# A spatial product of 768 x 768 computed from seven block products instead of eight

## The chip, the core and the metric

The kernel runs on one core of one Trainium2 chip. Its metric is the device time in microseconds of one execution. The core's engines run side by side, each through its own list of instructions, and meet at semaphores: TensorE (PE) multiplies into PSUM, VectorE (DVE) and ScalarE (ACT) work elementwise on SBUF and PSUM, GpSimd (POOL) works on SBUF, and SyncE (SP) issues nearly all DMAs.

## What is computed

A retention layer feeds an MLP with a low-rank token mixing, and that feeds a spatially gated MLP. The change is in the last part. Batch B is 2, sequence S is 768, model width 512, and all data are 32-bit.

```python
def _moe2_ref(x, w_in, w_spatial, b_spatial, w_out) -> np.ndarray:
    h = np.maximum(x @ w_in, 0.0)
    d_ff = h.shape[-1]
    u, v = (h[..., :d_ff // 2], h[..., d_ff // 2:])
    mu = np.mean(v, axis=-1, keepdims=True)
    var = np.mean((v - mu) ** 2, axis=-1, keepdims=True)
    v_n = (v - mu) / np.sqrt(var + 1e-06)
    v_s = np.einsum('ts,bsd->btd', w_spatial, v_n) + b_spatial[None, :, None]
    gated = u * v_s
    return (gated @ w_out).astype(np.float32)
```

## The kernel before

**Precision.** A 32-bit operand of a matrix product is split in two: ACT rounds it to fp32r (`vh`, `wsph`, `gh`, `x2h`, `wouth`), and DVE or POOL forms the rest, operand minus rounded part (`vl`, `wspl`, `gl`, `x2l`, `woutl`). PE then makes three matmuls for each pair of tiles: high times high, high times rest, rest times high.

**Stages.** The retention part takes the first 67 us. Then come the 24 steps of the MLP, n = 0 to 23 (three token tiles of 512, each with eight steps). Its first product (`product`) already uses a scheme of seven block products q = 0 to 6: sums of blocks are multiplied, and results are put together from PSUM and three copies p1, p16 and p5. From the second token tile on, the input projection (`in_first`, `in_group`) of the tile before runs inside the steps. That of the last tile, t = 2, comes by itself at 367 to 389 us; it waits for `x2h` and `x2l`, made from `u`, to which DVE adds the MLP's result (L848). Groups 0 to 3 of a token tile give V (`vn`, normalised over its 512 channels on DVE at L869 with statistics from L859 and L863 and POOL's `rstd`, L446). Groups 4 to 7 give u.

**The spatial part** has eight pieces m, four tiles of 128 channels d in each of two batches. For each piece PE multiplies the six row tiles of V (stationary, 128x128) with the six row tiles of w_sp (moving, two halves of 384 columns), three matmuls each: 36. DVE adds the bias (L986), multiplies with u (L989) into `gt`, ACT rounds it to `gh` (L683) and DVE forms `gl` (L992). After a batch's four pieces the output projection (`out_proj`, L1280) multiplies the four tiles of `gh` and `gl` with `wouth` and `woutl`. Four banks hold its results, which ACT copies to `stage` (L688) and SP stores. PE waits at `wout_lo` before the first one.

**What sets the order.** Each engine's list is written by hand, loop by loop, as the functions below show, and an engine goes through its list strictly in order; SP's DMAs are in one queue too. A semaphore counts finished operations, for instance `sp_done` pieces of the spatial product.

## Time and profile before

| | us |
|---|---|
| median of 3 runs | 477.98 (476.96 to 478.22) |
| the profiled execution | 477.27 |
| its span | 475.4 |
| PE busy | 466.1 |
| DVE busy | 318.2 |
| ACT busy | 233.0 |
| POOL busy | 53.7 |

The span runs from the first to the last instruction; the 1.9 us around it are start and end. All times in rows are in microseconds from the span's start unless marked ns. In a row of a timeline, an "x4" behind several merged instructions gives their number and the second column their common length; the brackets hold how long the engine was idle before and what ended it. A duration includes the time until the result is written, so the next instruction of the same engine starts some 0.1 us before the end of the one before it. The matmuls of PE overlap too: a start-to-start distance is their cost in a row, and the duration is a latency.

### The profile page before, as it was taken

Reading aid. Unit: us, or ns where it says so; the run is one execution under the profiler, and the core shown is the slowest. Engines: PE = TensorE matmul, PEld = TensorE weight load, DVE = VectorE, ACT = ScalarE, POOL = GpSimd, SP = SyncE. Lnnn points to the kernel's source line nnn. Section 1 sums busy time; section 2 is a strip of 40 time slices with the busy share of each in tenths; the row PEclk is TensorE's granted clock in tenths of the full one; section 3 lists DMA queues with packets and bytes.
Section 4 is the critical chain, followed back from the end, with each engine's and each line's share of the span. In section 5 each row is a group of like instructions: output and inputs, shape, how many; then the busy total and the mean of one; then the engine's idle time right before and its main releaser. Section 6 shows DMA issues by size and latency. Waiting matters only on the chain.

```text
span 475.4 us, 8542 instructions
## 1 busy us (share of the span) xinstructions
PE 466.1 (98%) x3176; PEld 417.4 (88%) x3176; DVE 318.2 (67%) x697; ACT 233.0 (49%) x540; POOL 53.7 (11%) x56
## 2 busy tenths in 40 slices
PE   7999998999999999999999999999999999999997
PEld 4788887989999999888888998888888889999997
DVE  4788978888789988764765977765633684611630
ACT  1666745555667655643474555643333732222112
POOL 2278960000000000000100000001000050000000
PEclk9999999999999999999999999999999999999999
DMA  8999801362222342211220432220115200011003
GB/s 270 413 314 305 280 1 45 135 221 88 90 89 90 128 138 91 90 50 38 90 90 10 135 123 90 90 70 21 44 29 209 84 0 1 1 68 66 1 0 134
DMA packets 19929, 50.31 MB, mean 106 GB/s; under 512 B 1456, under 2 KB 3120, under 8 KB 18608
## 3 DMA queue, kind: packets, MB, share of 16 engines
q1 hardware_dynamic: 19472, 49.24, 29.9%
q10 hardware_dynamic: 416, 0.53, 0.4%
q8 instruction: 26, 0.43, 0.4%
q14 instruction: 15, 0.12, 0.1%
HBM read 46.61 MB, written 3.15 MB: 105 GB/s over the span
## 4 chain that ended last, share of the span: by engine, by line
PE 93%; DVE 2%; DMA 2%; ACT 1%; issue 1%; SPq 0%; DVEq 0%
PE bank L1265 11%; PE bank L1177 9%; PE bank L1175 9%; PE bank L1178 9%; PE bank L1158 8%; PE bank L1156 8%; PE bank L1159 8%; PE bank L1280 7%; PE bank L1217 2%; PE bank L1216 2%; PE bank L1215 2%; PE bank L1025 2%; PE bank L1070 2%; PE bank L1064 2%; DMA att<-attn 1%; PE bank L1210 1%
## 5 line engine op out<-in xcount | busy, mean ns | idle before, releaser
L1156 PE MATMUL bank<-bh,w1c 128*128 128x256 f32 x336 | 94.7, 282 | 2.2 <-DVE c L830 0.8
L1159 PE MATMUL bank<-bh,w1c 128*128 128x256 f32 x336 | 94.7, 282 | 0.0
L1158 PE MATMUL bank<-bl,w1c 128*128 128x256 f32 x336 | 94.6, 282 | 0.0
L1177 PE MATMUL bank<-hl,w2h 128*128 128x512 f32 x192 | 75.9, 396 | 0.0
L1175 PE MATMUL bank<-hh,w2h 128*128 128x512 f32 x192 | 75.8, 395 | 0.0
L1178 PE MATMUL bank<-hh,w2l 128*128 128x512 f32 x192 | 74.7, 389 | 0.0
L1156 PEld LDWEIGHTS bank<-bh,w1c 128*128 128x128 f32 x336 | 63.5, 189 | 9.2 <-DVE w1c L797 2.8
L1158 PEld LDWEIGHTS bank<-bl,w1c 128*128 128x128 f32 x336 | 63.4, 189 | 5.5
L830 DVE TENSOR_TENSOR c<-bank,p 128x256 f32<-128x256 f32 x72 | 30.5, 424 | 52.1 <-PE bank L1159 31.0
L1159 PEld LDWEIGHTS bank<-bh,w1c 128*128 128x128 f32 x336 | 63.4, 189 | 0.0
L549 ACT ACTIVATE p<-bank 128x256 f32<-128x256 f32 x72 | 27.5, 381 | 47.0 <-PE bank L1159 46.0
L1178 PEld LDWEIGHTS bank<-hh,w2l 128*128 128x128 f32 x192 | 36.1, 188 | 7.9
L564 ACT ACTIVATE hh<-c 128x256 fp32r<-128x256 f32 (+1 forms) x48 | 25.1, 523 | 30.8 <-DVE c L830 30.8
L1177 PEld LDWEIGHTS bank<-hl,w2h 128*128 128x128 f32 x192 | 36.6, 191 | 2.1
L524 ACT ACTIVATE w1c<-wsum 128x256 fp32r<-128x256 f32 x96 | 35.2, 410 | 6.6 <-DVE wsum L789 4.7
L1175 PEld LDWEIGHTS bank<-hh,w2h 128*128 128x128 f32 x192 | 36.2, 188 | 2.4
L797 DVE TENSOR_TENSOR w1c<-wsum,w1c 128x256 fp32r<-128x256 f32 x92 | 36.5, 417 | 0.0
L802 DVE TENSOR_TENSOR w2l<-w2raw,w2h 128x512 fp32r<-128x512 f32 x46 | 31.4, 683 | 7.2 <-ACT w2h L541 7.2
L444 POOL TENSOR_SCALAR vare<-mv 128x4 f32<-128x4 f32 x3 | 0.7, 226 | 314.0 <-DVE mv L863 314.0
L541 ACT ACTIVATE w2h<-w2raw 128x512 fp32r<-128x512 f32 x48 | 29.8, 620 | 0.0
L986 DVE TENSOR_TENSOR gt<-bank,bias_sb 128x384 f32<-128x384 f32 x16 | 8.2, 553 | 31.4 <-PE bank L1265 31.4
L524 ACT ACTIVATE w1c<-w1raw 128x256 fp32r<-128x256 f32 x72 | 26.8, 406 | 1.7 <-DMA w1raw<-w 1.7
(120 smaller groups left out, 904.4 us busy)
## 6 DMA issues: line engine op xcount, KB each, us to landing
w1raw<-w SPq DMA_DIRECT2D x24, 512.0 KB, 5.0
w2raw<-w SPq DMA_DIRECT2D x24, 512.0 KB, 4.0
att<-attn SPq DMA_DIRECT2D x7, 1152.0 KB, 7.2
att<-attn SPq DMA_DIRECT2D x10, 384.0 KB, 5.3
out_T<-stage SPq DMA_DIRECT2D x7, 384.0 KB, 2.3
wsp_raw<-w_sp SPq DMA_DIRECT2D x1, 2304.0 KB, 8.2
winraw<-w_in SPq DMA_DIRECT2D x1, 2048.0 KB, 9.4
tab<-decay SPq DMA_DIRECT2D x7, 258.0 KB, 4.2
```

The costliest lines, as they stand in the source:

```text
L524: nc.scalar.activation(w1c[k][:, 0, q, :], w_operand(k, q), ACT.Copy).then_inc(w1_hi, 1)
L797: nc.vector.tensor_tensor(w1c[k][:, 1, q, :], w_operand(k, q), raw(w1c[k])[:, 0, q, :], ALU.subtract).then_inc(w1_lo, 1)
L802: nc.vector.tensor_tensor(w2l[h][:, :], w2raw[n % 2][:, h, :], raw(w2h[h])[:, :], ALU.subtract).then_inc(w2_lo, 1)
L830: nc.vector.tensor_tensor(o, b, a[:, :], ALU.add).then_inc(c_sum, 1)
L1156: mm(o, w1c[k][:, 0, q, s], bh[:, q, c, :], start=(opens and c == 0), stop=False, skip_group_check=True)
L1158: mm(o, w1c[k][:, 0, q, s], bl[:, q, c, :], start=False, stop=False, skip_group_check=True)
L1159: m = mm(o, w1c[k][:, 1, q, s], bh[:, q, c, :], start=False, stop=(c == 1), skip_group_check=True)
L1175: mm(ch_ps[c][:, :], w2h[h][:, s], hh[k][:, h, :], start=(j == 0 and h == 0), stop=False, skip_group_check=True)
L1177: mm(ch_ps[c][:, :], w2h[h][:, s], hl[k][:, h, :], start=False, stop=False, skip_group_check=True)
L1178: m = mm(ch_ps[c][:, :], w2l[h][:, s], hh[k][:, h, :], start=False, stop=last, skip_group_check=True)
L1265: i = mm(o[h], w[m % 2][:, s, :], x[:, s, h * HS:(h + 1) * HS], start=(first and s == 0), stop=(last and s == NC - 1))
L1280: i = mm(o[h], w[:, d, s], x[:, d, h * HS:(h + 1) * HS], start=(first and d == 0), stop=(last and d == CT - 1))
```

## The change

**PE.** The eight pieces become four blocks a (two per batch), each of two d tiles by the whole token range. V^T and w_sp are split into two halves each way: the two d tiles, the two halves of the summed rows (three tiles of 128 each), and the two halves of 384 output columns. Seven products of three row tiles with three matmuls each make a block, 63 matmuls. The products go into bank x, z, x, y, x, y, x in the order of q, where x alternates between two banks from block to block. x and y are not opened by a matmul: ACT writes the bias, or the difference of its halves, into them first (`set_bias`).

**DVE** forms sums of blocks of w_sp (`sums_wsp`, four of 1152 columns, then seven rests) and of V (`sums_v`, four of 384 for each block, then seven rests). Per block it makes three result sums (`sum_sp`), four gates that write in place into u (`gate`), and four rests, in place too. The statistics of the last token tile move from behind `rest_v(1)` into block 1, and their normalisation behind block 1.

**ACT** rounds seven operands for each block and seven for w_sp, copies p1s, p16s and p5s out of PSUM, and writes the biases. The rounding of w_out moves into block 1.

**SP** loads the bias in MLP step 3, behind w_in, and w_out behind the input projection. `stage` holds one batch instead of two.

**POOL** keeps its list.

The diff, cut to the lists of ACT, DVE, SP and PE:

```diff
-        vs_ps, out_ps = [bank[0:2], bank[2:4]], bank[4:8]
+        x_ps, z_ps, y2_ps, out_ps = bank[2:4], bank[0], bank[4], (bank[1], bank[5], bank[6], bank[7])
...
                 if n == 3:
                     sp.wait_ge(u_done, 2 * NI)
                     sp.dma_start(winraw[:, :, :], w_in).then_inc(win_loaded, 16)
+                    sp.dma_start(bias_sb[:, :], bias).then_inc(bias_loaded, 16)
             sp.wait_ge(pr_done, NQ * NN)
             sp.dma_start(wsp_raw[:, :, :], w_sp).then_inc(wsp_loaded, 16)
-            sp.dma_start(bias_sb[:, :], bias).then_inc(wsp_loaded, 16)
-            sp.wait_ge(ch2_done, 2 * NN)
+            sp.wait_ge(in_done, 8 * NT)
             sp.dma_start(woutraw[:, :, :], w_out).then_inc(wout_loaded, 16)
...
+            def set_bias(a, i):
+                if i == 0:
+                    if a == 0:
+                        act.wait_ge(bias_loaded, 16)
+                        act.wait_ge(x2_sum, 4 * NT)
+                    elif a == 1:
+                        act.wait_ge(x2_sum, 4 * NT)
+                    else:
+                        act.wait_ge(gated, 4 * (a - 1))
+                    nc.scalar.activation(x_ps[a % 2][:, 0:HS], bias_sb[:, 0:HS], ACT.Copy).then_inc(bias_set, 1)
+                else:
+                    if a == 0:
+                        act.wait_ge(diff_done, 1)
+                        act.wait_ge(x2_sum, 4 * NT)
+                    else:
+                        act.wait_ge(sp_sum, 3 * a)
+                    nc.scalar.activation(y2_ps[:, 0:HS], bias_diff[:, :], ACT.Copy).then_inc(bias_set, 1)
...
+            for a in range(NA):
+                sp_copy(a, 0)
+                if a:
+                    set_bias(a, 1)
+                if a == 0:
+                    round_v(1, range(0, 2))
+                round_g(a, 0)
+                sp_copy(a, 1)
+                if a == 0:
+                    round_v(1, range(2, 4))
+                sp_copy(a, 2)
+                if a == 0:
+                    round_v(1, range(4, NQ))
+                elif a == 1:
+                    round_wout()
+                round_g(a, 1)
+                round_g(a, 2)
+                if a < NA - 1:
+                    set_bias(a + 1, 0)
+                round_g(a, 3)
+                if a == 1:
+                    round_v(2, range(NQ))
+                    out_copy(0, 0)
+                    out_copy(0, 1)
+                    round_v(3, range(NQ))
+                    out_copy(0, 2)
+                    out_copy(0, 3)
...
+            sums_v(0)
+            rest_v(0, range(0, 2))
+            add_x2(NT - 1, range(0, 3))
+            rest_v(0, range(2, 4))
+            add_x2(NT - 1, range(3, 4))
             rest_x2(NT - 1)
...
-            rest_v(0)
-            rest_v(1)
-            statistics(NT - 1, range(CT))
-            normalise(NT - 1)
-            dve.wait_ge(in_out, 8 * NT)
-            for m in range(CT * B):
-                gate(m)
-                if m + 2 < CT * B:
-                    rest_v(m + 2)
+            bias_difference()
+            sums_wsp()
+            rest_v(0, range(4, NQ))
+            rest_wsp(range(NQ))
+            sums_v(1)
+            for a in range(NA):
+                sum_sp(a, 0)
+                gate(a, 0)
+                if a == 0:
+                    rest_v(1, range(0, 2))
+                elif a == 1:
+                    statistics(NT - 1, range(CT))
+                rest_g(a, 0)
+                sum_sp(a, 1)
+                gate(a, 1)
+                if a == 0:
+                    rest_v(1, range(2, 4))
+                sum_sp(a, 2)
+                gate(a, 2)
+                rest_g(a, 1)
+                if a == 0:
+                    rest_v(1, range(4, NQ))
+                gate(a, 3)
+                rest_g(a, 2)
+                rest_g(a, 3)
+                if a == 1:
+                    normalise(NT - 1)
+                    sums_v(2)
+                    rest_v(2, range(NQ))
+                    sums_v(3)
+                    rest_v(3, range(NQ))
...
+            def spatial(a):
+                k, x, z, y = a % 2, x_ps[a % 2][:, 0:HS], z_ps[:, 0:HS], y2_ps[:, 0:HS]
+                for q in range(NQ):
+                    o = (x, z, x, y, x, y, x)[q]
+                    if a == 0:
+                        pe.wait_ge(wsp_lo, q + 1)
+                    pe.wait_ge(vl_done, NQ * a + q + 1)
+                    if q == 0:
+                        pe.wait_ge(bias_set, 2 * a + 1)
+                    if q == 1 and a:
+                        pe.wait_ge(sp_sum, 3 * (a - 1) + 1)
+                    if q == 2:
+                        pe.wait_ge(sp_copied, 3 * a + 1)
+                    if q == 3:
+                        pe.wait_ge(bias_set, 2 * a + 2)
+                    if q == 4:
+                        pe.wait_ge(sp_copied, 3 * a + 2)
+                    if q == 5:
+                        pe.wait_ge(sp_copied, 3 * a + 3)
+                    if q == 6:
+                        pe.wait_ge(sp_sum, 3 * a + 2)
+                    for s in range(NH):
+                        mm(o, vh[k][q][:, s, :], wsph[:, q, s, :], start=(q == 1 and s == 0), stop=False,
+                           skip_group_check=True)
+                        mm(o, vh[k][q][:, s, :], wspl(q)[:, s, :], start=False, stop=False, skip_group_check=True)
+                        m = mm(o, v_rest(a, q)[:, s, :], wsph[:, q, s, :], start=False, stop=(s == NH - 1),
+                               skip_group_check=True)
+                    m.then_inc(sp_done, 1)
```

In POOL's list nothing moves. In DVE's list the piece around the last additions to u read so before (`u<-bank,u` is the addition, `w2l` the rest of the last w2 tile):

```order
532 L802 TENSOR_TENSOR w2l_88<-w2raw_84,w2h_87 128x512 [waits w2_hi]
533 L848 TENSOR_TENSOR u<-bank,u 128x512 [waits ch_sum] x3
534 L848 TENSOR_TENSOR u<-bank,u 128x512 [waits ch2_done]
535 L853 TENSOR_TENSOR x2l<-u,x2h 128x512 [waits x2_hi] x4
536 L970 TENSOR_TENSOR wspl<-wsp_raw,wsph 128x768 [waits wsp_hi] x6
```

and reads so now (`vsum` are sums of blocks of V, `vn_rest` and `vsum_rest` rests):

```order
532 L940 TENSOR_TENSOR w2l_88<-w2raw_84,w2h_87 128x512 [waits w2_hi]
533 L1121 TENSOR_TENSOR vsum_119<-vn 128x384 [waits hid_lo,vn_done]
534 L1121 TENSOR_TENSOR vsum_119<-vsum_119,vn 128x384 [waits v_sum]
535 L1121 TENSOR_TENSOR vsum_119<-vn 128x384
536 L1121 TENSOR_TENSOR vsum_119<-vn,vsum_119 128x384 [waits v_sum]
537 L1128 TENSOR_TENSOR vn_rest<-vn,vh_0_122 128x3x128 [waits vh_done,v_sum]
538 L1128 TENSOR_TENSOR vn_rest<-vn,vh_1_123 128x3x128 [waits vh_done]
539 L986 TENSOR_TENSOR u<-bank,u 128x512 [waits ch_sum] x3
540 L1128 TENSOR_TENSOR vsum_rest_141<-vsum_119,vh_2_124 128x384 [waits vh_done]
541 L1128 TENSOR_TENSOR vsum_rest_141<-vsum_119,vh_3_125 128x384 [waits vh_done]
542 L986 TENSOR_TENSOR u<-bank,u 128x512 [waits ch2_done]
543 L991 TENSOR_TENSOR x2l<-u,x2h 128x512 [waits x2_hi] x4
```

Six operations on V stand ahead of the additions and two more ahead of the fourth. The statistics of the last token tile (BN_STATS), for which POOL's `rstd` and then `woutl` wait, stood ahead of the first gate (L986) in DVE's list:

```order
538 L976 TENSOR_TENSOR vl_116<-vn,vh_115 128x768 [waits vh_done]
539 L859 BN_STATS bnst<-vn 128x6 [waits in_out]
540 L863 BN_AGGR mv<-bnst 128x2 [waits vn_done,bn_done]
541 L859 BN_STATS bnst<-vn 128x6 [waits in_out]
542 L863 BN_AGGR mv<-bnst 128x2 [waits vn_done,bn_done]
543 L859 BN_STATS bnst<-vn 128x6 [waits in_out]
544 L863 BN_AGGR mv<-bnst 128x2 [waits vn_done,bn_done]
545 L859 BN_STATS bnst<-vn 128x6 [waits in_out]
546 L863 BN_AGGR mv<-bnst 128x2 [waits vn_done,bn_done]
547 L869 TENSOR_SCALAR vn<-vn,mv,rstd 128x512 [waits rstd_done]
548 L869 TENSOR_SCALAR vn<-vn,mv,rstd 128x512 x3
549 L986 TENSOR_TENSOR gt_120<-bank,bias_sb 128x384 [waits sp_done,in_out]
```

They now stand in block 1 (`csum` is a result sum, `u<-csum,u` a gate, `u_rest` its rest):

```order
579 L1172 TENSOR_TENSOR u<-csum_115,u 128x384 [waits sp_sum]
580 L997 BN_STATS bnst<-vn 128x6 [waits in_out]
581 L1001 BN_AGGR mv<-bnst 128x2 [waits vn_done,bn_done]
582 L997 BN_STATS bnst<-vn 128x6 [waits in_out]
583 L1001 BN_AGGR mv<-bnst 128x2 [waits vn_done,bn_done]
584 L997 BN_STATS bnst<-vn 128x6 [waits in_out]
585 L1001 BN_AGGR mv<-bnst 128x2 [waits vn_done,bn_done]
586 L997 BN_STATS bnst<-vn 128x6 [waits in_out]
587 L1001 BN_AGGR mv<-bnst 128x2 [waits vn_done,bn_done]
588 L1176 TENSOR_TENSOR u_rest<-u,gh 128x384 [waits gh_done]
589 L1161 TENSOR_TENSOR csum_114<-bank,p5s 128x384 [waits gated,sp_done,sp_copied]
590 L1172 TENSOR_TENSOR u<-csum_114,u 128x384 [waits sp_sum]
```

Eight rows of statistics stand between the gate and the rest of block 1's first quarter, behind the whole of block 0. ACT's list read so before, beside the first three pieces (`vh` a rounding of V, `gh` one of the gated tile):

```order
433 L678 ACTIVATE vh_113<-vn 128x768 [waits sp_done]
434 L683 ACTIVATE gh<-gt_120 128x768 [waits gated]
435 L678 ACTIVATE vh_115<-vn 128x768 [waits sp_done]
436 L683 ACTIVATE gh<-gt_121 128x768 [waits gated]
437 L678 ACTIVATE vh_113<-vn 128x768 [waits sp_done,vn_done]
```

The end of block 0 and the start of block 1 read now:

```order
451 L746 ACTIVATE vh_6_135<-vn 128x384
452 L786 ACTIVATE gh<-u 128x384 [waits gated] x2
453 L764 ACTIVATE bank<-bias_sb 128x384 [waits x2_sum]
454 L786 ACTIVATE gh<-u 128x384 [waits gated]
455 L780 ACTIVATE p1s<-bank 128x384 [waits sp_sum,sp_done]
456 L771 ACTIVATE bank<-bias_diff 128x384 [waits sp_sum]
457 L786 ACTIVATE gh<-u 128x384 [waits gated]
```

Row 453 writes the bias for block 1's first product. It stands behind the second and third rounding of the gated tile (L786) of block 0. Before, ACT wrote nothing that a spatial matmul's bank waited for.

## Rows read from the trace of the kernel before

**Rows 1.** The page: engine shares; granted clock in 40 slices, in tenths.

```profile
PE 466.1 (98%) x3176; PEld 417.4 (88%) x3176; DVE 318.2 (67%) x697; ACT 233.0 (49%) x540; POOL 53.7 (11%) x56
...
PEclk9999999999999999999999999999999999999999
```

**Rows 2.** The longest wait of PE in the table of waits; the chain in order.

```profile
PE bank L1103 <- DVE hh L714: 1.4, 1, 1.4
...
389.00 24.98 PE bank L1265 x144
413.99 16.66 PE bank L1280 x96
```

**Rows 3.** Timeline at the spatial part; groups of instructions (busy, mean ns).

```profile
388.84 0.51 PE L1265 MATMUL bank<-wsph,vh 128*128 128x384 f32 x2
...
401.54 1.02 DVE L986 TENSOR_TENSOR gt<-bank,bias_sb 128x384 f32<-128x384 f32 x2 [1.41 <-PE bank L1265]
...
L541 ACT ACTIVATE w2h<-w2raw 128x512 fp32r<-128x512 f32 x48 | 29.8, 620 | 0.0
...
L693 ACT ACTIVATE wsph<-wsp_raw 128x768 fp32r<-128x768 f32 x6 | 4.8, 836 | 0.0
L688 ACT ACTIVATE stage<-bank 128x384 f32<-128x384 f32 x16 | 7.1, 490 | 21.6 <-PE bank L1280 21.6
```

**Rows 4.** MLP step 3: SP's issue of w_in, its time to landing; ACT; PE.

```profile
89.62 0.60 SPq L362 DMA_DIRECT2D winraw<-w_in  x1
...
winraw<-w_in SPq DMA_DIRECT2D x1, 2048.0 KB, 9.4
...
100.34 0.72 ACT L524 ACTIVATE w1c<-w1raw 128x256 fp32r<-128x256 f32 x2 [1.70 <-DMA w1raw<-w]
100.97 0.36 ACT L549 ACTIVATE p<-bank 128x256 f32<-128x256 f32 x1
...
101.77 0.28 PE L1156 MATMUL bank<-bh,w1c 128*128 128x256 f32 x1
```

**Rows 5.** Timeline where the last input projection begins: DVE, ACT, PE.

```profile
362.90 0.69 DVE L802 TENSOR_TENSOR w2l<-w2raw,w2h 128x512 fp32r<-128x512 f32 x1 [7.18 <-ACT w2h L541]
365.15 2.73 DVE L848 TENSOR_TENSOR u<-bank,u 128x512 f32<-128x512 f32 x4 [1.56 <-PE bank L1178]
...
365.87 2.67 ACT L571 ACTIVATE x2h<-u 128x512 fp32r<-128x512 f32 x4 [3.01 <-DVE u L848]
371.72 0.60 ACT L577 ACTIVATE vn<-bank 128x512 f32<-128x512 f32 x1 [0.97 <-PE bank L1201]
...
366.99 0.39 PE L1194 MATMUL bank<-winh,x2h 128*128 128x512 f32 x1
...
372.71 0.39 PE L1211 MATMUL bank<-winl,x2h 128*128 128x512 f32 x1
```

**Rows 6.** Timeline of DVE and POOL from the last statistics to woutl.

```profile
381.27 0.69 DVE L859 BATCH_NORM_STATS2 bnst<-vn 128x6 f32<-128x512 f32 x1
...
384.37 0.18 DVE L863 BATCH_NORM_AGGREGATE mv<-bnst 128x2 f32<-128x6 f32 x1
386.03 5.80 DVE L869 TENSOR_SCALAR vn<-vn,mv,rstd 128x512 f32<-128x512 f32 x4 [1.47 <-POOL rstd L446]
...
384.95 1.04 POOL L446 TENSOR_TENSOR rstd<-vare,neg_half 128x4 f32<-128x4 f32 x1
385.96 5.58 POOL L469 TENSOR_TENSOR woutl<-woutraw,wouth 128x512 fp32r<-128x512 f32 x4
```

**Rows 7.** Timeline of POOL and DVE: a DVE operation alone and meeting POOL's.

```profile
55.85 2.52 POOL L429 TENSOR_TENSOR bl<-u,bh 128x512 fp32r<-128x512 f32 x2
58.33 1.87 POOL L429 TENSOR_TENSOR bl<-tsum_early,bh 128x512 fp32r<-128x512 f32 x1
...
57.34 1.72 DVE L752 TENSOR_TENSOR qd<-att,tab 128x640 f32<-128x640 f32 x1
...
13.30 0.83 DVE L752 TENSOR_TENSOR qd<-att,tab 128x640 f32<-128x640 f32 x1 [0.88 <-DMA tab<-decay]
```

More of the change, by code:

```diff
@@ L147, in retention_mlp_spatial_gating_kernel @@
-        woutraw, o = at("woutraw", W2_AT, [P, CT, C])
-        wouth, o = at("wouth", o, [P, CT, C], f32r)
-        woutl, o = at("woutl", o, [P, CT, C], f32r)
-        assert o <= C_AT
-        o = C_AT
-        for k in range(2):
-            gt[k], o = at(f"gt{k}", o, [P, S])
+        stage, o = at("stage", o, [P, CT, S])
+        wouth, o = at("wouth", o, [P, CT, C], f32r)
+        assert o <= VN_AT
+        woutraw, o = at("woutraw", VN_AT + 24 * KB, [P, CT, C])
+        p1s, o = at("p1s", o, [P, HS])
@@ new lines, in retention_mlp_spatial_gating_kernel @@
+        p16s, o = at("p16s", o, [P, HS])
+        p5s, o = at("p5s", o, [P, HS])
+        csum = [None, None]
+        for k in range(2):
+            csum[k], o = at(f"csum{k}", o, [P, HS])
+        assert o <= U_AT
+        wsp_raw, o = at("wsp_raw", B_AT, [P, NC, S])
+        wt, o = at("wt", o, [P, 4, NH, HS])
+        wsph, o = at("wsph", o, [P, NQ, NH, HS], f32r)
+        assert o <= W2R_AT
+        vsum, vh = [None, None], [[None] * NQ for _ in range(2)]
+        vsum[0], o = at("vsum0", C_AT, [P, 4, NH, P])
@@ L681, in round_g, with round_v @@
-            def round_g(m):
-                act.wait_ge(gated, m + 1)
-                nc.scalar.activation(gh[:, m % CT, :], gt[m % 2][:, :], ACT.Copy).then_inc(gh_done, 1)
+            def round_v(a, qs):
+                b, k = a // 2, a % 2
+                for q in qs:
+                    if q == 0:
+                        act.wait_ge(vn_done, CT * (b + 2))
+                        act.wait_ge(ch2_done, 2 * (NN - 1 + a) if a < 2 else 2 * NN)
+                    if q == 5 and a < 2:
+                        act.wait_ge(w2_lo, 2 * NN - 4 + 2 * a)
+                    if q in S_OF:
+                        act.wait_ge(v_sum, 4 * a + S_OF[q] + 1)
+                    if a >= 2:
+                        act.wait_ge(sp_done, NQ * (a - 2) + q + 1)
+                    nc.scalar.activation(vh[k][q][:, :, :], v_operand(a, q), ACT.Copy).then_inc(vh_done, 1)
@@ L685, in out_copy, with round_wout @@
+            def round_wout():
+                act.wait_ge(wout_loaded, 16)
+                for d in range(CT):
+                    nc.scalar.activation(wouth[:, d, :], woutraw[:, d, :], ACT.Copy).then_inc(wout_hi, 1)
             def out_copy(b, c):
+                if b:
+                    act.wait_ge(stage_free[c], 16)
                 for h in range(2):
                     act.wait_ge(out_done, 8 * b + 2 * c + h + 1)
-                    nc.scalar.activation(stage[:, c, b * S + h * HS:b * S + (h + 1) * HS],
+                    nc.scalar.activation(stage[:, c, h * HS:(h + 1) * HS],
@@ L701, in _ @@
[L701 to L709 removed]
+            round_v(0, range(NQ))
+            round_x2(NT - 1, range(CT))
+            set_bias(0, 0)
+            round_wsp(0)
+            round_wsp(1)
+            relu_in(NT - 1, range(0, 2))
@@ L712, in _ @@
+            for c in range(CT):
+                out_copy(1, c)
         @block.vector
@@ new lines, in sum_sp, with gate @@
+            def sum_sp(a, s):
+                copied, q, p, ps = ((1, 1, p1s, z_ps), (3, 4, p5s, x_ps[a % 2]), (2, 5, p16s, y2_ps))[s]
+                dve.wait_ge(sp_copied, 3 * a + copied)
+                dve.wait_ge(sp_done, NQ * a + q + 1)
+                k = 3 * a + s
+                if k >= 2:
+                    dve.wait_ge(gated, 4 * ((k - 2) // 3) + (k - 2) % 3 + 1)
+                nc.vector.tensor_tensor(csum[k % 2][:, :], ps[:, 0:HS], p[:, :], ALU.add).then_inc(sp_sum, 1)
+            def gate(a, s):
+                if s < 3:
+                    dve.wait_ge(sp_sum, 3 * a + s + 1)
+                    x = csum[(3 * a + s) % 2][:, :]
+                else:
+                    dve.wait_ge(sp_done, NQ * (a + 1))
+                    x = x_ps[a % 2][:, 0:HS]
+                if a == 0 and s == 0:
+                    dve.wait_ge(in_out, 8 * NT)
+                nc.vector.tensor_tensor(u_part(u, a, s), x, u_part(u, a, s), ALU.mult).then_inc(gated, 1)
@@ L1285, in _ @@
             for b in range(B):
-                for d in range(CT):
-                    spatial(CT * b + d)
+                spatial(2 * b)
+                spatial(2 * b + 1)
                 if b == 0:
```

225 lines of the change are left out of this document (142 added, 83 removed).

## The prediction

> **What bounds the kernel now.** I read the engine shares first: PE is busy for 98% of the span, at the full granted clock in all forty slices [rows 1]. So the question is whether PE's queue has holes where the change works. The chain in order of time says no: the first four spatial pieces are one unbroken run of 24.98 us, and the first output projection is one of 16.66 us right behind it [rows 2]. The longest wait of PE that the table of waits shows is 1.4 us, at the start [rows 2]. Here every matmul taken away is time gained and every wait put in is time lost, to the full.
>
> The spatial part is 288 matmuls of 384 columns. 144 of them are the run of 24.98 us [rows 2]: 0.1735 us each. From a last matmul's start to the start of DVE or ACT is 0.39 us: the run begins at 388.84, its 72nd matmul at 388.84 + 71 x 0.1735 = 401.16, DVE starts at 401.54 [rows 3].
>
> **What goes.** Four blocks of seven products of nine matmuls are 252 instead of 288. 36 x 0.1735 = **6.25 us less** on PE. Each matmul still has a weight load of its own before and after, and the single bank per product costs nothing: the last output matmuls and the MLP's products already accumulate into one.
>
> **What is added, by place.** For 384 columns I take on DVE 0.55 us to the end and 0.47 to the next start, from the pair of 1.02 us out of PSUM [rows 3]; 0.83 us for 640 columns in SBUF [rows 7] is the same rate. On ACT I take 0.52 and 0.42, between 0.49 out of PSUM and the line through 0.62 for 512 and 0.84 for 768 columns in SBUF [rows 3]. Wider ones go by the same slopes: 1152 columns cost DVE 1.27 and ACT 1.05. Waking PE costs 0.17 more: the copy freed its bank at 372.32 and the matmul that was due at 372.43 has its successor at 372.71 [rows 5].
>
> *1. The bias load, moved ahead of a weight load.* SP now issues it between w_in and the fifth w1 tile. That tile was the one DMA that ACT waited for (1.70 us, until 100.34), with the copy p16 queued behind it on ACT; the copy ended at 101.33 and PE's fifth product started at 101.77 [rows 4]. So the cover is 101.77 - 101.33 - 0.17 = 0.27 us. w_in landed at 89.62 + 9.4 = 99.0 and the tile's 512 KB behind it at 100.3, so 384 KB more are 1.0 us: PE stands for 1.0 - 0.27 = **0.75 us** (0.3 if the DMA engines have room, 1.1 without cover).
>
> *2. The first V sums, ahead of the last x2 adds.* Before, DVE ended the last rest of w2, waited 1.56 us and started adding at 365.15; ACT rounded from 365.87 and PE started on it at 366.99 without a hole [rows 5]. Now DVE has, from 362.90 + 0.60 = 363.50, four sums (0.58, 0.47, 0.47, 0.58 with the waits on its own results) and two rests (0.94): the adds start at 366.53, 1.38 late. ACT's seven roundings end inside that. The first x2h is then ready at 367.88 and PE starts at 368.05, 1.06 late. Two more rests in front of the fourth add put it at 369.26, the last x2 rest ends at 372.35 and PE's matmul on its tile loses 0.15. ACT then has the bias write and two roundings of 1152 columns (1.05 each) before the first ReLU: 0.1 more. **1.3 us** (1.1 to 1.5). The wsp sums and rests behind it (4 x 1.27 and 7 x 1.27 us on DVE) end at 388.3, under the input projection, which ends at 390.1.
>
> *3. Between block 0 and 1.* I count from a block's first matmul; a product is 1.56 us, a block 10.93. ACT writes the next block's bias behind two roundings of the gated tile, though its bank has been free for long. Fifth product done 8.03; DVE sum 8.03, gate 8.61, two rests of V until 10.02; sum for C12 10.02, gate 10.60, ACT's rounding 11.19, bias write 11.61 to 12.10; PE 12.27. **1.35 us** (1.1 to 1.6). An ACT write from SBUF into PSUM has no row here; I take the 0.49 of a copy out of PSUM, the nearest, with 0.4 and 0.6 as ends.
>
> *4. Block 1, and the weights of the output projection.* This is the largest term. PE waits for all four woutl tiles before the projection. Before, POOL made them at 385.96 to 391.5, twenty-two microseconds ahead of need [rows 6]. Now POOL comes to them behind rstd, which waits for DVE's statistics of the last token tile, which stand between the first gate and its rest in block 1. In block time: first gate 3.92, statistics 4.38 to 7.68 (3.28 us, from 381.27 to 384.55 [rows 6]), variance 8.1, rstd 8.45 to 9.45 (1.04 [rows 6]), then four rests. Alone they take 1.24 each (2.52 for two [rows 7]): done at 14.1, a stall of 3.3 us. That is the lower end, because POOL and DVE get in each other's way when both read SBUF: DVE's qd took 0.83 us alone and 1.72 when it met a POOL operation, which itself ended at 60.20 after 1.87 instead of 1.28; and DVE's normalisation ran at 1.45 per tile beside POOL (5.80 for four) [rows 6, 7]. So each blocks the other for an instruction. In block 1 the gates and rests with both inputs in SBUF meet POOL's chain four times, and each time POOL stands for about 0.4 us: first rest 9.87, second 11.5, third 13.15, fourth 14.85 to 16.1. PE starts at 16.3 instead of 10.93: **5.3 us** (3.3 to 5.7). The activations' own rests are in time: for the third d tile 14.9, for the fourth 16.7, needed 2.1 and 6.2 us behind the start.
>
> The 0.4 is scaled from the row: POOL lost 1.87 - 1.28 = 0.59 to an instruction of 0.83, which is 0.39 for one of 0.55. The Trainium skill (SBUF — State Buffer, "Who interferes with whom") calls the shared ports an exclusive lock, held for the whole instruction. By that each meeting would cost POOL the full 0.55 and this term would be 5.9; the row says less, and I keep to the row.
>
> *5. Between block 2 and 3.* As 3 without V's rests: sum 9.59, gate 10.17, rounding 10.76, bias write 11.18 to 11.67, PE 11.84: **0.9 us** (0.7 to 1.1).
>
> *At no cost.* The copies p1, p16, p5 and the sums inside a block are due 1.56 us after the product that they follow and need 0.39 + 0.5 to 1.1; the tightest is the second sum of block 1, behind the statistics, done at 8.7 for 9.37 (slack 0.5 with the wake-up). The late w_out load, 1 MB from 390, would take some 5 us by w_in's 2 MB in 9.4 and is needed 18 us later. Stores through one half-sized staging tile: the second batch's first copy comes 30 us behind the first batch's store. The second half of V is normalised from about 419 and rounded by 427; PE needs it at 435. The tail after the last matmul is as before.
>
> **Sum.** -6.25 + 0.75 + 1.3 + 1.35 + 5.3 + 0.9 = **+3.35 us**. The profiled execution took 477.27 (span 475.4): 480.6. Its time is 0.7 below the median of the runs shown, 477.98, from which it would be 481.3. I give 480.9. With all ends low the sum is +0.3, with all high +4.8; the four small terms vary apart, so 478.4 to 482.5 for this case.
>
> **Rivals.**
> *The clock falls in the long wait.* PE would stand for 5 us, where nothing in the trace is longer than 1.4, and the granted clock was 1.00 throughout, the 2.4 GHz level. If it falls to 1.2 GHz, a 384-column matmul takes about twice 0.1735. If that lasts as long as the wait did, an assumption, 5.3 us of queue have half the rate and 2.6 us are lost: 483.5. For it: the wait is nearly four times the longest seen. Against: dense work on both sides. The Trainium skill (TensorE: Matmul & The Clock Gate, "Loop structure matters more than you think") has PE go cold when it waits between matmuls; no row here tests it.
> *POOL is not held up.* If the two engines rarely meet and the hand-offs are at their low ends, the sum is 3.3 + 0.4 + 1.1 + 1.1 + 0.7 - 6.25 = +0.35: 477.6 to 478.3, no difference.
> *Faster: the four woutl tiles are in time.* If POOL had rstd and the tiles done by 10.8 in block 1, term 4 is gone: -6.25 + 4.3 = -1.95, 475.7. It needs POOL to take the tiles' 5 us before the statistics are done, against its order, or PE to reach block 1's end 3.3 us later than the product count says. I see nothing for it.
> *The hand-offs inside a block don't fit.* If the copy behind a product came 1.0 us later than walked, each of some twelve of them would cost about 0.2: +2.4, 483.3. The MLP's products, with the same copies, run without holes, which speaks against it.
>
> **Chances.** A measurement of this kernel tells 0.3%, 1.43 us, from no change. The forecast case has 0.62, the clock 0.14, no hold-up 0.12, hand-offs 0.07, faster 0.05. Of the forecast case one part in ten lies within 1.43 us of no change. So faster 0.05, same 0.17, slower 0.78. The range 478.2 to 483.6 leaves out the faster case, part of the no hold-up case and the tops of the others.
>
> **What would show it.** A hole of PE of about 5 us before the first output projection, released by POOL's woutl; its length is term 4. Spatial matmuls 252, at 0.1735. Holes of 1.3 and 0.9 us at the first matmuls of block 1 and 3, released by ACT's bias write. The first input-projection matmul of the last tile 1 us late behind DVE's u. An ACT wait of 2.7 instead of 1.7 us for the fifth w1 tile. Wrong would be: woutl ready before block 1 ends, or the granted clock under 1.00 behind the hole.

## The result and the profile after

| | before | after |
|---|---|---|
| median, us | 477.47 (476.71 to 478.22, 4 runs) | 484.16 (483.34 to 486.45, 4 runs) |
| the profiled execution, us | 477.27 | 483.38 |
| its span, us | 475.4 | 481.5 |

The ratio is 1.0142, 95% interval 1.0116 to 1.0168: the changed kernel is 6.7 us slower, where the forecast was 480.9 and the range ended at 483.6. The direction was right and the time was outside the range. A second series gave 483.24 (481.35 to 484.71, 6 runs) beside 478.30, ratio 1.0104 (1.0076 to 1.0131).

The page of the kernel after, its first lines: PE's share fell from 98% to 96%, and its busy line has an 8 and a 6 in the thirty-fourth and thirty-fifth slice. The clock's line says 9 everywhere, as before, because the short low stretch shown below is spread over two slices of 12 us.

```profile
span 481.5 us, 8647 instructions
PE 464.1 (96%) x3140; PEld 412.9 (86%) x3140; DVE 339.5 (71%) x751; ACT 251.7 (52%) x589; POOL 54.3 (11%) x56
PE   8999998989999999999999999999999998699997
PEclk9999999999999999999999999999999999999999
```

PE's busy line of the kernel before:

```profile
PE   7999998999999999999999999999999999999997
```

The table of PE's waits of the kernel after (line that waited, line that released it, us in total, times, longest). In before its first line was a wait of 1.4 us [rows 2].

```profile
PE bank L1508 <- POOL woutl L535: 4.2, 1, 4.2
PE bank L1368 <- ACT p L615: 2.5, 2, 1.9
PE bank L1489 <- ACT bank L764: 2.0, 2, 1.2
PE bank L1315 <- DVE hh L852: 1.4, 1, 1.4
PE bank L1368 <- DVE c L968: 0.8, 1, 0.8
PE bank L1406 <- ACT x2h L637: 0.8, 1, 0.8
```

The first three and the sixth are new or grown, and each is at a place that the prediction named. Timelines of PE, kernel after: the first matmul behind each of these waits, in order of time, and behind the wait for woutl the first pairs of the output projection.

```profile
104.13 0.36 PE L1368 MATMUL bank<-bh,w1c 128*128 128x256 f32 x1 [1.88 <-ACT p L615]
370.40 0.50 PE L1406 MATMUL bank<-winh,x2h 128*128 128x512 f32 x1 [0.81 <-ACT x2h L637]
404.93 0.41 PE L1489 MATMUL bank<-wsph,vh 128*128 128x384 f32 x1 [1.22 <-ACT bank L764]
420.35 1.01 PE L1508 MATMUL bank<-gh,wouth 128*128 128x384 f32 x2 [4.23 <-POOL woutl L535]
421.16 0.84 PE L1508 MATMUL bank<-u_rest,wouth 128*128 128x384 f32 x2
421.80 0.84 PE L1508 MATMUL bank<-gh,woutl 128*128 128x384 f32 x2
450.43 0.41 PE L1489 MATMUL bank<-wsph,vh 128*128 128x384 f32 x1 [0.76 <-ACT bank L764]
```

The pairs behind 420.35 are 0.81 and 0.64 us apart; at the rate of before (16.66 us for 96, [rows 2]) a pair takes 0.35. The chain in order of time, kernel after, has the two output projections as unbroken runs; the first one took 18.39 us where before had 16.66.

```profile
420.35 18.39 PE bank L1508 x96
461.59 16.74 PE bank L1508 x96
```

The clock is why, as the first experiment shows. The table of stretches, kernel after (us, PE busy, PEld, DVE, ACT, POOL with their instructions, granted clock, DMA share, GB/s):

```profile
416.00:420.30 4.30, 0.12 (x1) 0.00 (x0) 4.30 (x5) 1.43 (x3) 4.30 (x3) 0.98 0.00 0
420.30:423.00 2.70, 2.65 (x8) 2.65 (x9) 2.67 (x6) 0.42 (x1) 0.00 (x0) 0.50 0.00 0
423.00:425.00 2.00, 2.00 (x11) 2.00 (x11) 1.93 (x5) 1.76 (x5) 0.00 (x0) 0.86 0.00 0
425.00:437.00 12.00, 12.00 (x71) 11.93 (x70) 8.40 (x18) 6.46 (x16) 0.00 (x0) 1.00 0.25 95
```

The 0.98 is a mean: the clock stood at 1.00 until 420.1 and fell some 0.2 us before PE began again. PE then ran at 0.50, the 1.2 GHz level, and the clock was back at the 2.4 GHz level at 423.5; the 0.86 is the mean of a stretch with both levels.

**The account**, each term as the shift of PE's matmuls against before:

| term | forecast | measured |
|---|---|---|
| 36 matmuls fewer | -6.25 | -6.25 |
| start of the kernel, unchanged code | 0 | +0.3 |
| 1. bias load | +0.75 | +0.6 |
| w_in lands later in this execution | none | +1.5 |
| 2. V sums ahead of the x2 additions | +1.3 | +1.3 |
| 3. block 0 to 1 | +1.35 | +1.5 |
| 4. wait for woutl | +5.3 | +4.4 |
| the clock behind it | none | +1.7 |
| 5. block 2 to 3 | +0.9 | +1.0 |
| sum | +3.35 | +6.05 |

The spans differ by 6.1. PE's fifth product of step 3 began at 104.13, and before at 101.77 [rows 4]; less the shift at the start that is 2.1. Its division into 0.6 and 1.5 is worked out from the profiles of the bias load below, with the load counted first, so that it gets the cover of 0.27; counted last it would be 0.9 for the load and 1.2 for w_in. Term 3 is the gap of 1.22 plus what the woken matmul starts late; term 4 is 420.35 less the end of block 1 at 415.96.

### The profile page after: what moved, and what is told of

The parts are those of the page before. It is cut to its first block, busy times and chain, and to the rows that moved or that the text cites. A ratio compares the mean times of both kernels' runs of the same rounds, so it can differ in the third digit from the quotient of the medians.

```text
span 481.5 us, 8647 instructions
## 1 busy us (share of the span) xinstructions
PE 464.1 (96%) x3140; PEld 412.9 (86%) x3140; DVE 339.5 (71%) x751; ACT 251.7 (52%) x589; POOL 54.3 (11%) x56
## 4 chain that ended last, share of the span: by engine, by line
PE 85%; DMA 5%; DVE 4%; issue 1%; POOL 1%; ACT 1%; SPq 0%; POOLq 0%; DVEq 0%; ACTq 0%
PE bank L1389 8%; PE bank L1387 8%; PE bank L1390 8%; PE bank L1368 8%; PE bank L1370 8%; PE bank L1371 8%; PE bank L1508 7%; DMA w1raw<-w 2%; PE bank L1489 2%; PE bank L1492 2%; PE bank L1491 2%; PE bank L1429 2%; PE bank L1428 2%; PE bank L1427 2%; PE bank L1237 2%; PE bank L1282 2%
## 5 line engine op out<-in xcount | busy, mean ns | idle before, releaser
L1489 PE MATMUL bank<-wsph,vh 128*128 128x384 f32 x84 | 28.2, 336 | 2.0 <-ACT bank L764 2.0
## 6 DMA issues: line engine op xcount, KB each, us to landing
winraw<-w_in SPq DMA_DIRECT2D x1, 2048.0 KB, 10.9
```

The source lines that it names most:

```text
L1489: mm(o, vh[k][q][:, s, :], wsph[:, q, s, :], start=(q == 1 and s == 0), stop=False, skip_group_check=True)
```

## The experiments

The theory: (a) the wait for woutl comes from POOL's queue, lengthened by DVE and POOL shutting each other out; (b) the clock falls behind that wait and costs 1.7 us; (c) the bias load, put ahead of a weight load, costs 2 us, for instance because it also makes w_in in front of it land later; (d) the other terms are the hand-offs as walked. The rivals stand in the expectations. The kernels with the extra matmuls, the earlier statistics, the bias load back and the early load in before share 15 runs of before (median 478.10); those with the late load, the bias write, the V rests and everything together share 16 (478.76); the kernel with DVE and POOL apart and the repeated one share 11 (478.30). After has two medians, 484.16 and 483.24, and both are given where a kernel is set against it.

### The clock: 24 matmuls without use in the hole

```
+ for _ in range(24):
+     mm(out_ps[3][:, 0:HS], vh[1][0][:, 0, :], wsph[:, 0, 0, :], start=True, stop=True,
+        skip_group_check=True)
  pe.wait_ge(wout_lo, CT)
```

> The kernel after with 24 extra matmuls of 384 columns (4.2 us of work, into a bank that the projection opens anew) ahead of PE's wait for woutl, so PE is busy in the hole of 4.4 us that the trace after shows. Theory: the first output projection took 18.4 instead of 16.7 us because the granted clock was at half when PE came back; with PE kept busy the clock stays at 1.00 from 416 to 425 us, the projection takes 16.7 and the kernel is 1.7 us faster, up to 3 in executions with a longer low stretch. Rival: the projection is slow because DVE, ACT and POOL work beside it; then it stays at 18.4 and the time is unchanged or slightly longer.

Measured: 481.22 (480.59 to 482.58, 5 runs), ratio 1.0067 (1.0043 to 1.0091), span 479.4. The stretches of this kernel, over the same window:

```profile
416.00:420.30 4.30, 4.15 (x24) 3.83 (x23) 4.30 (x5) 0.73 (x2) 3.54 (x3) 1.00 0.00 0
420.30:423.00 2.70, 2.70 (x17) 2.70 (x16) 2.63 (x7) 0.94 (x2) 0.00 (x0) 1.00 0.03 6
```

The same tiles are awaited, DVE and POOL do the same, and with PE kept at work the clock stays at 1.00: in 420.3 to 423 there are 17 matmuls instead of 8. The mean clock of all five runs is 0.999 or more, of the ten runs of after 0.993 or 0.996. That the clock falls because PE stood, and what this costs, is shown. The first output projection took 16.95 us from its first to its last matmul, 1.4 less than in after. The rival, a projection slowed by the engines beside it, is refuted: they work beside it here too. The medians are 2.9 and 2.0 us below those of after. In the two profiles the spans differ by 2.1: 1.4 is the projection, the rest was there before block 0, w_in having landed after 9.3 us instead of 10.9. Half of the runs of after also have a second fall of the clock (below), and none of these five has.

### POOL and DVE: statistics earlier

```
  sums_v(1)
+ statistics(NT - 1, range(CT))
  for a in range(NA):
...
- elif a == 1:
-     statistics(NT - 1, range(CT))
```

ACT's rounding of w_out is moved with it into block 0 (two tiles behind each of two roundings).

> The kernel after with the statistics of the last token tile ahead of block 0, in DVE's idle 3.2 us there, and the rounding of w_out in ACT's gaps of block 0. Theory: the hole before the first output projection (4.4 us) is due to POOL's list, which starts at the end of the statistics; it goes, and with it the low clock behind it (1.7 us): 6.1 us faster than the kernel after, about 478. Rival: woutl then meets DVE's gates in block 0 and 1 and delays them, so the hole moves to the starts of block 1 and the gain is 3 to 4.

Measured: 484.81 (481.19 to 485.45, 4 runs), ratio 1.0114 (1.0063 to 1.0165). The wait for woutl is gone from the output projection and has a substitute a block earlier. Timelines of POOL, DVE and PE of this kernel:

```profile
403.21 5.92 POOL L535 TENSOR_TENSOR woutl<-woutraw,wouth 128x512 fp32r<-128x512 f32 x4 [3.99 <-ACT wouth L791]
403.46 1.46 DVE L1173 TENSOR_TENSOR u<-csum,u 128x384 f32<-128x384 f32 x1
404.84 3.17 DVE L1129 TENSOR_TENSOR vsum_rest<-vsum,vh 128x384 fp32r<-128x384 f32 x2
407.93 0.54 DVE L1162 TENSOR_TENSOR csum<-bank,p16s 128x384 f32<-128x384 f32 x1
410.63 0.66 PE L1489 MATMUL bank<-wsph,vh 128*128 128x384 f32 x1 [5.10 <-ACT bank L764]
```

DVE's gate took 1.46 instead of 0.56 us, and two rests 3.17 instead of 1.02, while POOL made its tiles. Block 0 ends with a chain of sum, gate and rounding ahead of the next bias write. Counted from the block's start it is now 3.4 us late at the sum and 3.9 at the bias write. The operation in the middle that reads PSUM kept its 0.54. So beside the four tiles DVE lost 3.5 us (0.9, 2.15, and 0.5 in the gate behind the sum) and POOL 1.0, and moving the tiles into another block moves the hole.

The theory's 6.1 us did not come, and neither did the 3 to 4 us of the rival, whose mechanism this is: the medians are 0.7 above the first series of after and 1.6 above the second. In the profile the granted clock was 0.50 from 408.4 to 415.3, which lengthened block 1 by 2.2 us. With the 3.9 of the moved hole that uses up what the woutl wait and its low clock had cost. A further fall, in MLP step 3, cost 1.6.

### POOL and DVE apart

```
  gate(a, 2)
+ if a == 1:
+     gate(a, 3)
+     dve.wait_ge(wout_lo, CT)
  rest_g(a, 1)
...
- gate(a, 3)
+ if a != 1:
+     gate(a, 3)
```

> After, but in block 1 DVE does its last gate first and makes its last three rests of the gated tile only when POOL has finished the four woutl tiles. Theory (the two engines shut each other out when both work in SBUF): the tiles met a sum's gate and two or three of these rests; with the rests gone only the gate of 0.56 us is left, so the four take 5.2 to 5.4 us instead of 5.91, the rests take 0.55 each instead of 1.62 and 2.69 for two, and PE's wait for the tiles is 0.5 to 0.7 us shorter (about 3.6). Rival (POOL's four tiles take 5.9 us by themselves): no change of POOL's row and the same wait of 4.2. The clock falls behind the wait in either case. Time: 0.6 below the repeated kernel after by the theory, none by the rival; too small for the rounds, so the rows decide.

Measured: 483.73 (481.34 to 484.83, 4 runs), 1.0104 (1.0072 to 1.0136). POOL and DVE of the kernel after, and behind them of this one:

```profile
414.39 5.91 POOL L535 TENSOR_TENSOR woutl<-woutraw,wouth 128x512 fp32r<-128x512 f32 x4
416.02 1.62 DVE L1176 TENSOR_TENSOR u_rest<-u,gh 128x384 fp32r<-128x384 f32 x1
418.03 2.69 DVE L1176 TENSOR_TENSOR u_rest<-u,gh 128x384 fp32r<-128x384 f32 x2
```

```profile
416.31 5.26 POOL L535 TENSOR_TENSOR woutl<-woutraw,wouth 128x512 fp32r<-128x512 f32 x4
417.16 0.85 DVE L1172 TENSOR_TENSOR u<-csum,u 128x384 f32<-128x384 f32 x1
421.61 1.49 DVE L1176 TENSOR_TENSOR u_rest<-u,gh 128x384 fp32r<-128x384 f32 x3 [2.97 <-POOL woutl L535]
PE bank L1512 <- POOL woutl L535: 3.6, 1, 3.6
```

With one gate as DVE's only operation with both inputs in SBUF beside it, POOL makes the four tiles in 5.26 us; with three rests beside it as well, in 5.91. The three rests alone take 1.49 together, beside POOL 4.31. PE's wait is 3.6 instead of 4.2. The theory's numbers are met. What remains, 3.6 us of the wait, is POOL's queue, with the statistics and `rstd` in front. The time did not follow (the repeated after has 483.24). In the profiled execution the clock also fell in MLP step 3, and two of these four runs have that second fall, so a few tenths can't be read off these medians.

### The bias load

The load goes back behind that of w_sp:

```
- sp.dma_start(bias_sb[:, :], bias).then_inc(bias_loaded, 16)
  sp.dma_start(wsp_raw[:, :, :], w_sp).then_inc(wsp_loaded, 16)
+ sp.dma_start(bias_sb[:, :], bias).then_inc(bias_loaded, 16)
```

> The kernel after with one edit: the bias load is issued behind the load of w_sp, where the kernel before has it. Theory: the trace after shows the fifth w1 tile landing at 102.96 instead of 100.34 us and PE 2.1 us further behind at the fifth product of MLP step 3; without the bias load in front ACT's wait for that tile is back at 1.7 us and the whole is 2.1 us faster than the kernel after. Rival: the late tile is scatter of the DMA engines in one execution; then the bias costs what the 384 KB cost by bytes, about 0.8 us, and the tile lands late now and then in every kernel.

Measured: 481.45 (480.6 to 483.53, 5 runs), 1.0072 (1.0043 to 1.0102), 2.7 and 1.8 us below the two series of after. ACT's wait was 2.8 us and PE's 0.7; w_in landed after 10.6 us. Two of the five runs have a mean clock of 0.993, a second fall without the early load. The other way round, only this load is moved ahead in the kernel before:

> The kernel before with one edit, the early bias load behind w_in. Theory: the load alone costs what it cost in the kernel after, 2.1 us, since nothing else of the change touches MLP step 3. Rival: 0.75 us, the cost by bytes that was forecast, with the rest of the 2.1 us due to something else in the kernel after.

Measured: 481.09 (477.77 to 482.83, 10 runs), 1.0055 (1.0029 to 1.0081), 3.0 above before, more than the theory's 2.1. ACT's row and PE's in the kernel before with the early load:

```profile
102.81 0.72 ACT L525 ACTIVATE w1c<-w1raw 128x256 fp32r<-128x256 f32 x2 [3.93 <-DMA w1raw<-w]
103.95 0.36 PE L1158 MATMUL bank<-bh,w1c 128*128 128x256 f32 x1 [1.78 <-ACT p L550]
```

The wait that was 1.70 [rows 4] is 3.93, and PE stands for 1.8 us. The ten runs fall into two groups: four have a mean clock of 1.000 and times of 477.8 to 479.5, six have 0.996 and 480.7 to 482.8. With the early load alone the clock falls in more than half of these executions; of the 42 runs of before beside the experiments it did in 4. The profile is one of the four without a fall.

A third position, behind the fifth w1 tile:

```
+ if n == 4:
+     sp.dma_start(bias_sb[:, :], bias).then_inc(bias_loaded, 16)
```

> The kernel after with the bias load issued behind the fifth w1 tile instead of ahead of it. Theory: what costs is standing ahead of that tile in SP's queue, so the tile lands as without the bias load (wait of ACT 1.7 to 2.8 us, PE's extra wait at the fifth product of step 3 0 to 0.8 us) and the time is that of the kernel with the bias load back at w_sp, 481.5 within 0.8. Rival: the extra DMA traffic itself slows w_in and the tile; then ACT waits 3.9 us as in the kernel after and the time is 483 to 485.

Measured: 482.55 (481.82 to 483.53, 6 runs), 1.0083 (1.0056 to 1.0111). The median is 0.2 us above what the theory gave, the wait with 3.3 us 0.5 above. Three kernels with the load far behind had waits of 1.7, 2.3 and 2.8, and their w_in had landed after 9.4, 10.1 and 10.6 us: the wait grows with w_in's landing, one for one. What was open was whether the bias load makes w_in late. Before and before with the early load were profiled again, in turn on one chip:

> Before with the early bias load, one more profile. Over the profiles so far ACT's wait for the fifth w1 tile is 1.7 + (landing of w_in - 9.4), and 0.9 more with the bias load ahead of the tile. If the load also delays w_in (theory): w_in 10.6 to 11.2 and a wait of 3.8 to 4.4. If w_in's landing is scatter (rival): anywhere from 9.3 to 11.2, with a wait of 2.5 to 4.4 by the same line.

> Before, one more profile. Theory: w_in at 9.3 to 10.2 and a wait of 1.6 to 2.5. Rival: 9.3 to 11.2, wait 1.6 to 3.5 by the same line.

> As the first look with the early load: theory w_in 10.6 to 11.2, wait 3.8 to 4.4; rival 9.3 to 11.2.

> As the first look at before: theory w_in 9.3 to 10.2, wait 1.6 to 2.5; rival 9.3 to 11.2.

They took 477.4, 478.5, 479.58 and 478.46 us, one run each, all at a mean clock of 1.000. ACT's row and PE's, first in the first new profile of the kernel before, and then in the first new one with the early load:

```profile
101.78 0.72 ACT L524 ACTIVATE w1c<-w1raw 128x256 fp32r<-128x256 f32 x2 [3.58 <-DMA w1raw<-w]
102.92 0.36 PE L1156 MATMUL bank<-bh,w1c 128*128 128x256 f32 x1 [1.43 <-ACT p L549]
```

```profile
100.70 0.72 ACT L525 ACTIVATE w1c<-w1raw 128x256 fp32r<-128x256 f32 x2 [2.40 <-DMA w1raw<-w]
101.84 0.36 PE L1158 MATMUL bank<-bh,w1c 128*128 128x256 f32 x1 [0.25 <-ACT p L550]
```

All profiles by the position of the load:

| bias load | w_in lands after, us | ACT's wait, us | PE's, us |
|---|---|---|---|
| far behind | 9.4, 10.1, 10.6, 10.8, 11.3 | 1.7, 2.3, 2.8, 3.0, 3.6 | 0, 0.2, 0.7, 0.8, 1.4 |
| behind the w1 tile | 11.0 | 3.3 | 1.1 |
| ahead of the w1 tile, w_in early | 9.2, 9.3, 9.5 | 2.4, 2.5, 2.7 | 0.25, 0.3, 0.6 |
| ahead of the w1 tile, w_in late | 10.7 to 11.2 (seven) | 3.9 to 4.3 | 1.8 to 2.2 |

The rival is right. w_in scatters by 2 us from one execution to the next, in the kernel before as well. The wait is 1.7 plus what w_in lands beyond 9.4, and 0.8 to 0.9 more with the early load; behind the tile the load costs nothing. So the load's own price is 0.8 to 0.9 of the wait, near the 1.0 forecast, and the profile of before on record happened to be the earliest landing of its kernel. The late landing hits before and after alike, but only with the load on top does PE's wait reach 1.8 to 2.2 us. In two of the seven such profiles, those of the earlier statistics and of DVE and POOL apart, the clock fell right behind it, and from there to block 0 PE took 290.0 us instead of 288.5 in after: 1.6 us for the fall.

That such falls are a part of the 3.0 us is shown by the mean clock of the six slower runs. That they lay in MLP step 3 there is not shown, since no profile caught one; and the two groups' medians, 479.3 and 481.9, differ by more than a fall costs. The early load isn't needed for a fall either: besides the 4 of 42 runs of before, two of five with the load back and one of six with the late load have one more than the fall behind woutl.

### The bias write between blocks

```
  if a:
      set_bias(a, 1)
+ if a < NA - 1:
+     set_bias(a + 1, 0)
...
- if a < NA - 1:
-     set_bias(a + 1, 0)
  round_g(a, 3)
```

> The kernel after with one edit: ACT writes the next block's bias right behind its first copy in the block instead of behind the third rounding. Theory: the holes of PE at the start of block 1 (1.4 us) and block 3 (1.0 us) go, 2.4 us in all. Rival: DVE's rests of V, which follow the gates, hold PE next, so the hole of block 1 is only shortened, and what PE gains in block 1 it loses in a longer wait for woutl, whose start hangs on DVE's statistics: net gain 1.0.

Measured: 480.79 (479.06 to 484.1, 10 runs), 1.0057 (1.0026 to 1.0087), 3.4 and 2.5 below the two series of after. No wait on the bias write is left; inside block 1 there is 0.4 us on the copy p1s. So terms 3 and 5 were the write's place in ACT's queue, behind the rounding of the gated tile. In the profiles block 1 starts 1.4 us and block 3 0.9 earlier, counted from the block before, and of the 1.4 some 0.3 goes again up to the output projection: 2.0 of the theory's 2.4. The rest of the difference in this profile is w_in, landed after 9.5 us.

### The sums ahead of the additions

On DVE the rests of V go behind the x2 additions, on ACT three of the seven roundings behind those of x2 (only DVE's edit is shown):

```
  sums_v(0)
- rest_v(0, range(0, 2))
- add_x2(NT - 1, range(0, 3))
- rest_v(0, range(2, 4))
- add_x2(NT - 1, range(3, 4))
+ add_x2(NT - 1, range(CT))
...
- rest_v(0, range(4, NQ))
+ rest_v(0, range(NQ))
```

> The kernel after with the rests of V's first block moved behind the additions to u and their rests, on DVE, and three of seven roundings behind those of x2 on ACT; the four sums stay ahead. Theory: the last input projection starts 0.1 instead of 1.1 us late and has no further wait for x2l or the first ReLU: 1.2 us faster than the kernel after. Rival: the moved rests and roundings are then late for the spatial product or hold the ReLUs, and the gain is under 0.5.

Measured: 483.33 (482.8 to 485.03, 4 runs), 1.0106 (1.006 to 1.0151). The span is 480.8, 0.7 below after, where the theory had 1.2. The wait at 370.4 is gone, with 0.3 us left further on, and from MLP step 3 to block 0 PE gained 0.8. Nothing is lost behind that: PE's wait of 1.2 us at the start of block 1 is put down to a V rest instead of the bias write, but it is as long as in after, and block 1 starts 12.3 us behind block 0 in both. Of term 2 some 0.6 us stays; half of it is the 0.3, the other half was not traced.

### All of these together

Bias load back, bias writes early, V rests behind the additions, statistics before block 0, and w_out rounded at the start of block 1, not in block 0, so that POOL's tiles fall where DVE has slack.

> The kernel after with all waits attacked together: bias load behind w_sp, the next block's bias written early, the head order of the run before this one, the statistics ahead of block 0, and w_out rounded at the start of block 1, so that POOL makes woutl from some 2.7 to 9 us in block 1. Theory: only the 6.25 us of removed matmuls are left, less some 0.5 us of small waits: 5.5 to 6 us faster than the kernel before, about 472, granted clock 1.00. Rival: woutl still ends after block 1 because DVE and POOL hold each other up there, or DVE's gates come late for the seventh product: a hole of 1 to 3 us, 473 to 476.

Measured: **474.21 us (473.31 to 474.93, 5 runs), ratio 0.9909 (0.9874 to 0.9943)**, span 471.4: faster than both kernels. Its table of waits, POOL's row, and the first output projection:

```profile
PE bank L1486 <- ACT p1s L780: 0.8, 1, 0.8
PE bank L1486 <- ACT p16s L780: 0.3, 1, 0.3
PE bank L1419 <- ACT vn L643: 0.3, 1, 0.3
405.63 5.34 POOL L535 TENSOR_TENSOR woutl<-woutraw,wouth 128x512 fp32r<-128x512 f32 x4 [10.89 <-ACT wouth L791]
412.99 16.66 PE bank L1505 x96
```

POOL is done at 411.0, two microseconds ahead of need. The projection is at the rate of before, 16.66 us, and the mean clock of all five runs is 0.999 or more. Of the 6.25 us that the scheme takes away, 4.5 are left between the medians. That lies above the theory's 472 and in the range of its rival, but the rival's hole at woutl isn't there. The largest loss is inside block 1: from the first spatial matmul at 389.28 to the projection at 412.83 PE took 23.55 us, where 126 matmuls at 0.1735 are 21.86, and the waits for the copies p1s and p16s above are most of these 1.7 us.

### The kernel after once more

> The changed kernel again, for more runs: 483 to 486.5 us by all theories, ratio to before 1.011 to 1.017. The question is how far the landing of w_in, and with it ACT's wait for the fifth w1 tile, moves from one execution to the next: 4.0 us at its first run; if 2.3 to 4.0 with no edit, the scatter of 0.5 to 1.7 us seen between the experiments is not of their edits.

Measured: 483.24 (481.35 to 484.71, 6 runs). ACT's wait was 4.05 us, PE's 1.9 there and 4.2 for woutl, as in the first profile, so this pair doesn't show the scatter that it was to bring out. Half of the ten runs of after have a mean clock of 0.996 and took 481.35 to 483.38; the other half have 0.993 and took 483.19 to 486.45. The fall behind the wait for woutl is in both profiles, each with a mean of 0.996; a mean of 0.993 is one fall more. Where that lies in these five runs no profile shows.

## Why the prediction came out as it did

**PE bounds the kernel, and every matmul and wait counts in full.** Right. The measured terms add up to the difference of the spans within 0.1 us, and the combined kernel gave back most of what the waits had taken.

**What goes, -6.25.** Right: 252 spatial matmuls, and runs in a block at 0.17 from start to start.

**Term 1, the bias load, 0.75.** Right for the load itself: 0.9 of ACT's wait less the cover of 0.27, some 0.6 for PE. What failed is that the working took the landing of w_in (9.4 us) as fixed. It was the earliest of the five profiles with the load far behind, so the cover of 0.27 mostly isn't there, and the base, 477.27, was 0.8 to 1.5 below the medians of the 42 further runs of before (478.1, 478.76 and 478.3). And the longer wait that results has a fall of the clock of its own in part of the executions, which the sum didn't have.

**Term 2, 1.3.** Right in place and size (1.33, the growth of PE's shift over the first matmuls of the last input projection).

**Terms 3 and 5, 1.35 and 0.9.** Right (1.5 and 1.0). The write of ACT from SBUF into PSUM took 0.48 us, between my ends of 0.4 and 0.6.

**Term 4, 5.3.** The mechanism is right, the size 0.9 too high, in the range. POOL's `rstd` ended at 414.4 as walked. The walk had four meetings with DVE at 0.4 us each; POOL lost 0.95 over four tiles (5.91 for 4 x 1.24): three of them took 1.6 us, 0.3 more than the first, and none lost more. DVE lost more: 1.62 for a rest of 0.55. The Trainium skill (SBUF — State Buffer, "Who interferes with whom") has an exclusive lock for the whole instruction. The stretched rows go with it: a rest of 1.62 is 0.55 plus 1.07, nearly one tile of POOL's 1.24. But my reading, that POOL pays a full instruction of DVE at every meeting and the term would be 5.9, does not.

**The clock.** This is the step that failed most: the forecast case put nothing in the sum for it, and its rival had a chance of 0.14. "Dense work on both sides" was the reason against it, and it didn't protect here: the clock fell to 0.50 behind the hole with PE busy before and after it. The rival's price was 2.6 us and the measured one 1.7, as the low clock lasted 3.4 us, to 423.5, and not the 5.3 us of the wait that was forecast. The rule of the Trainium skill that I named beside this rival (TensorE: Matmul & The Clock Gate, "Loop structure matters more than you think") was right, and the trace now agrees: granted clock 0.50 behind a single wait of 4.2 us. With it, the measured terms and 0.9 for a bias load without cover the same sum is -6.25 + 0.9 + 1.3 + 1.5 + 4.4 + 1.7 + 1.0 = +4.55 for executions of one fall, and +6.15 with the 1.6 of a second one, which half of them have. The two series gave 4.9 and 6.7; the 6.7 is taken from a before of 477.47, which is 0.6 to 1.3 below the later medians of before, and how far that difference is chance stays open.

**The other rivals.** POOL not held up, woutl in time, and hand-offs that don't fit all fell with the measurements: block 0 had no wait inside, and blocks 1 to 3 had none but at their starts.

## What to carry to other kernels

On a kernel whose PE never rests, price a new wait of several microseconds with the clock that falls behind it as a part of the forecast case, not as a rival. What takes work off PE also takes away the time that hid the other engines' chains: look at what each engine has in its queue in front of what PE needs next (here the statistics before woutl, the rounding before a bias write), and place work that is free early, such as a constant write, in front. Keep POOL's tiles apart in time from DVE's operations that take all their tiles from SBUF, or both pay; and don't put a transfer that is needed much later ahead of one that an engine waits for.

## What was not expected of the hardware

- Behind a wait of only 1.8 to 2.2 us the clock fell too, in some executions and not in others. Stretches of MLP step 3, in the kernel with DVE and POOL apart and then in the kernel after, repeated:

```profile
96.00:110.00 14.00, 11.83 (x66) 10.41 (x65) 8.27 (x22) 5.28 (x14) 0.00 (x0) 0.88 0.59 221
```

```profile
96.00:110.00 14.00, 12.10 (x77) 10.69 (x76) 10.04 (x24) 6.73 (x17) 0.00 (x0) 1.00 0.46 166
```

  PE was busy for 11.83 and 12.10 us, the waits were 2.2 and 1.9, and one has 66 matmuls, the other 77. What decides between them stays open: of seven profiles with a wait of 1.8 to 2.2 us two show a fall behind it. In all eight with a wait of 3.6 to 5.1 us the clock fell in it or behind it.
- The landing of the same 2 MB load ranged from 9.2 to 11.3 us between executions, with or without another load behind it. What sets it was not found.
- In these kernels DVE lost more to POOL than POOL to DVE: rests that take 0.55 alone took 1.62 and, two together, 2.69 and 3.17, while POOL's tiles went from 1.24 to 1.48 each on average. An operation with one large tile from SBUF was stretched too: DVE's normalisation of four tiles took 5.80 us beside POOL's tiles in before [rows 6] and 1.91 in after, with POOL idle. An operation of DVE that reads PSUM was not touched (0.54 in the midst of POOL's tiles).
